# Between two layers of a fused kernel: the routing count, the sums and the list of places reordered, three lists moved behind a weight split, filler transposes added

## The reference

```
attn = softmax(scale * q @ k.T, blocks of 64 causal) @ v        # 4 batches, 8 heads, 576 positions, 64 wide
x    = elu(x @ w_in) @ w_out                                    # 512 -> 2048 -> 512
do_compute = x @ w_skip > 0                                     # the others leave the kernel as x
e_idx  = argmax(x @ w_gate)                                     # one expert of 8 for each token
gate_w = softmax(x @ w_gate)[e_idx]
out[do_compute] = x + gate_w * (relu(x @ w1[e_idx]) @ w2[e_idx])   # 512 -> 1024 -> 512
```

## Time and profile before

| | |
|---|---|
| median of three runs | 790.11 us |
| profiled execution, its own time | 791.72 us |
| its span | 789.9 us |
| TensorE busy | 758.0 us, 96% of the span |
| VectorE, ScalarE, GpSimd busy | 66%, 44%, 31% |
| the chain that ended last: TensorE, ScalarE, VectorE | 86%, 5%, 4% |
| mean granted TensorE clock | 0.993 of full |

### The profile page before, as it was taken

The page is one execution under the profiler, slowest core; times in us unless marked ns, Lnnn a source line. Parts: engine busy times, 40 slices in busy tenths (PEclk is TensorE's granted clock), DMA queues, the critical chain, the costliest instruction groups (busy, mean ns, idle before and its releaser), DMA issues.

```text
span 789.9 us, 15565 instructions
## 1 busy us (share of the span) xinstructions
PE 758.0 (96%) x5170; PEld 639.8 (81%) x5171; DVE 524.1 (66%) x1331; ACT 347.8 (44%) x830; POOL 245.3 (31%) x240
## 2 busy tenths in 40 slices
PE   5999999899999999999999999999987999999995
PEld 3777777688998888898988998888865777887884
DVE  3888888954337974984797598436665997367342
ACT  3888888644322213223222322324452774446231
POOL 4888887944501201210121021000112231222211
PEclk9999999999999999999999999999998999999998
DMA  9556677462422112101210200502424898174000
GB/s 163 133 149 157 163 162 188 144 198 61 147 79 103 48 57 91 50 21 62 59 41 0 90 22 27 214 0 81 135 95 126 270 340 303 46 229 153 34 15 9
DMA packets 101061, 88.15 MB, mean 112 GB/s; under 512 B 63812, under 2 KB 78532, under 8 KB 100880
## 3 DMA queue, kind: packets, MB, share of 16 engines
q1 hardware_dynamic: 95584, 81.89, 34.7%
q0 software_dynamic: 3056, 5.00, 1.9%
q10 hardware_dynamic: 2368, 0.59, 0.4%
HBM read 72.26 MB, written 18.34 MB: 115 GB/s over the span
## 4 chain that ended last, share of the span: by engine, by line
PE 86%; ACT 5%; DVE 4%; issue 3%; DVEq 1%; DMA 1%; POOL 0%; SPq 0%; ACTq 0%; POOLq 0%
PE h_ps L1733 12%; PE out_ps L1733 12%; PE h_ps L1734 12%; PE h_ps L1735 12%; PE out_ps L1735 11%; PE out_ps L1734 11%; PE o_ps L684 5%; PE s_ps L668 3%; ACT prob L541 3%; PE t_ps L593 2%; PE out_ps L1869 1%; PE s_ps L663 1%; ACT pt L525 1%; PE tr_ps L1834 1%; DMA raw_qk<-in_q_dram 1%
## 5 line engine op out<-in xcount | busy, mean ns | idle before, releaser
L1558 ACT ACTIVATE ex<-h_ps 128x384 f32<-128x384 f32 x96 | 47.3, 493 | 272.3 <-PE h_ps L1735 272.3
L1733 PE MATMUL h_ps<-xt_hi,wi_hi 128*128 128x384 f32 x384 | 131.8, 343 | 0.0
L1734 PE MATMUL h_ps<-xt_lo,wi_hi 128*128 128x384 f32 x384 | 129.7, 338 | 0.0
L1735 PE MATMUL h_ps<-xt_hi,wi_lo 128*128 128x384 f32 x384 | 129.7, 338 | 0.0
L1394 DVE TENSOR_SCALAR ex<-ex 128x384 f32<-128x384 f32 x96 | 36.9, 385 | 131.1 <-ACT ex L1558 129.7
L1733 PE MATMUL out_ps<-wo_hi,gt 128*128 128x512 f32 x288 | 114.5, 398 | 0.0
L1735 PE MATMUL out_ps<-wo_hi,gt 128*128 128x512 f32 x288 | 113.9, 396 | 0.0
L1734 PE MATMUL out_ps<-wo_lo,gt 128*128 128x512 f32 x288 | 113.3, 393 | 0.0
L541 ACT ACTIVATE prob<-s_ps,negmax 128x128 f32<-128x128 f32 (+2 forms) x144 | 77.8, 556 | 14.1 <-DVE negmax L399 13.7
L1276 DVE CUSTOM_DVE_ANT_0 x2t<-x,w_raw 128x512 bf16<-128x512 f32 x108 | 82.7, 806 | 0.4
L1172 POOL TENSOR_TENSOR xt_lo<-x_raw,xt_hi 128x384 fp32r<-128x384 f32 x20 | 28.3, 1413 | 157.8 <-ACT xt_hi L1575 157.5
(11 more groups left out here) (180 smaller groups left out, 1589.0 us busy)
## 6 DMA issues: line engine op xcount, KB each, us to landing
w_raw<-in_moe_w_dram SPq DMA_DIRECT2D x56, 512.0 KB, 5.2
raw_qk<-in_q_dram SPq DMA_DIRECT2D x32, 144.0 KB, 3.2
attn_t<-attn_sb SPq DMA_DIRECT2D x16, 288.0 KB, 2.2
x_raw<-attn_t SPq DMA_DIRECT2D x24, 192.0 KB, 2.4
w_raw<-recip_rows SPq DMA_DIRECT2D x48, 96.0 KB, 2.8
out_dram<-x SPq DMA_DIRECT2D x18, 256.0 KB, 2.1
x_rows<-x SPq DMA_DIRECT2D x18, 256.0 KB, 2.6
v<-in_v_dram SPq DMA_DIRECT2D x32, 128.0 KB, 2.9
```

The source lines that it names most:

```text
L1558: act.activation(ex[:, f % 2], h_ps[:, f % 2, 0:NB], ACT.Exp).then_inc(ex_done, 1)
L1733: pe.matmul(dst, stat[0], mov[0], start=start, stop=False, skip_group_check=True)
L1734: pe.matmul(dst, stat[0], mov[1], start=False, stop=False, skip_group_check=True)
L1735: return pe.matmul(dst, stat[1], mov[0], start=False, stop=stop, skip_group_check=True)
```

## The change

- `assign`: the wait for the softmax sum, `guarded` and the reciprocal move behind both steps of `whole`.
- ScalarE's `soften(LAST, 2)` moves ahead of `relu(0, 0)`.
- The count is issued after six of the twelve matmuls of `hidden(0, 0, 0, 1)`.
- Two steps that copied the count and added the early shift become one; `memset` and seven one-element sums become three sums of eight elements, over a zeroed and padded row `sums`.
- The four loads of `meta_sb` stand between the two `ht_low`.
- The lists of experts 5, 6 and 7 move behind `now(1)`, `xt_low(1)` and the four `w1_low`.
- The gathers of tiles 0 and 1 take their offsets from `tile_ids`; `gather_ids` is not written for them.
- TensorE: six of eight chunks of `output(0, 0)`, 18 transposes of the identity into `lg_ps` (which nobody reads any more), `turn_x(1)`, and then the other two chunks.

The core of the diff:

```diff
-        META_STEPS = 6 + E - 1
+        META_STEPS = 7
@@ gather
-                hold(pool, held)
-                pool.tensor_copy(gather_ids[:, :], tile_ids[:, bass.ds(t, 1)]).then_inc(gather_set, 1)
+                known = isinstance(t, int) and t < 2
+                if known:
+                    pool.sem_inc(gather_set, 1)
+                else:
+                    hold(pool, held)
+                    pool.tensor_copy(gather_ids[:, :], tile_ids[:, bass.ds(t, 1)]).then_inc(gather_set, 1)
...
+                ids = tile_ids[:, t:t + 1].bitcast(U32) if known else gather_ids[:, 0:1]
@@ VectorE, first(e, i, t, ask)
                     past(0)
-                    for j in range(HALVES):
-                        ht_low(0, j)
+                    ht_low(0, 0)
                     at = [0] + [tiles_of(dve, listing)[0] for listing in range(1, E // 2 + 1)]
+                    ht_low(0, 1)
                     dve.wait_ge(table_in, 16)
-                    for listing in range(E):
-                        list_tiles(listing, at[listing] if listing < len(at) else tiles_of(dve, listing)[0])
+                    for listing in range(len(at)):
+                        list_tiles(listing, at[listing])
                     now(1)
                     xt_low(1)
                     for j in range(PIECES):
                         w1_low(1, 1, j)
+                    for listing in range(len(at), E):
+                        list_tiles(listing, tiles_of(dve, listing)[0])
@@ VectorE, the sums
-            chain(dve.tensor_copy(more_f[:, :], cnt))
-            chain(dve.tensor_tensor(more_f[:, 0:1], more_f[:, 0:1], base_e[0:1, 0:1], ALU.add))
+            more = sums[:, 0, PAD + 1:PAD + 1 + E]
+            dve.wait_ge(sums_zeroed, 3)
+            chain(dve.tensor_tensor(more_f[:, :], cnt, early_row[:, :], ALU.add))
             chain(dve.tensor_tensor(over[:, :, :], more_f[:, :].unsqueeze(2).to_broadcast([1, E, NT]),
                                     bound[:, :].unsqueeze(1).to_broadcast([1, E, NT]), ALU.is_gt))
-            chain(dve.tensor_reduce(more_f[:, :], over[:, :, :], AX_X, ALU.add))
-            chain(dve.memset(before_f[:, 0:1], 0.0))
-            for e in range(1, E):
-                chain(dve.tensor_tensor(before_f[:, e:e + 1], before_f[:, e - 1:e],
-                                        more_f[:, e - 1:e], ALU.add))
+            chain(dve.tensor_reduce(more, over[:, :, :], AX_X, ALU.add))
+            for step_at, by in enumerate((1, 2, 4)):
...
+                chain(dve.tensor_tensor(dst, row_in[:, PAD:PAD + E], row_in[:, PAD - by:PAD - by + E], ALU.add))
@@ ScalarE
+            soften(LAST, 2)
             relu(0, 0)
-            soften(LAST, 2)
@@ TensorE, first(e, i, t, ask)
-                    output(0, 0, range(FCE))
+                    output(0, 0, range(FCE - 2))
+                    for c in range(WARM):
+                        pe.transpose(lg_ps[:, 0:P], ident[:, :], ident[:, :])
                     turn_x(1)
+                    output(0, 0, range(FCE - 2, FCE))
@@ TensorE, ahead of the experts
-            hidden(0, 0, 0, 1)
+            hidden(0, 0, 0, 1, [0, 1])
             count(NT, rk_done)
+            hidden(0, 0, 0, 1, [2, 3])
```

More of the change, by code:

```diff
@@ L768, in experts @@
     HALVES = FE // BANK
+    WARM = 18
     TURN_K = 2
@@ L894, in experts @@
         before_f = sb("before_f", [1, E], F32)
+        PAD = E // 2
+        sums = sb("sums", [1, 3, PAD + E + 1], F32)
+        early_row = sb("early_row", [1, E], F32)
         meta_sb = sb("meta_sb", [1, E], I32)
@@ L940, in experts @@
         early_in, early_listed = sem("early_in"), sem("early_listed")
+        sums_zeroed = sem("sums_zeroed")
         table_in = sem("table_in")
@@ L1190, in gather @@
                     pool.wait_ge(listed, lists)
-                hold(pool, held)
-                pool.tensor_copy(gather_ids[:, :], tile_ids[:, bass.ds(t, 1)]).then_inc(gather_set, 1)
+                known = isinstance(t, int) and t < 2
[4 more added lines that the diff above has]
+                    pool.tensor_copy(gather_ids[:, :], tile_ids[:, bass.ds(t, 1)]).then_inc(gather_set, 1)
                 if is_zero(t):
                     pool.wait_ge(in_zeroed, 1)
-                if isinstance(t, int) and t < 2:
+                if known:
                     for s in range(TB):
@@ L1200, in gather @@
                 rows = LAST * NB if is_zero(t) else N
+                ids = tile_ids[:, t:t + 1].bitcast(U32) if known else gather_ids[:, 0:1]
                 pool.indirect_dma_start(
-                    e_in, None, x2_rows[0:rows, :], bass.IndirectOffsetOnAxis(ap=gather_ids[:, 0:1], axis=0),
+                    e_in, None, x2_rows[0:rows, :], bass.IndirectOffsetOnAxis(ap=ids, axis=0),
                     bounds_check=rows - 1, oob_is_err=False).then_inc(gathered, 16)
@@ L1338, in assign @@
                                   chosen[:, :], ALU.add).then_inc(route, 1)
-                made(t, A_STEPS + 3)
+                made(t, A_STEPS + 2)
                 dve.tensor_scalar(whole[:, :], slot_f[:, :], 1.0 / P, 0.5 / P - 0.5, ALU.mult,
                                   ALU.add).then_inc(route, 1)
-                dve.reciprocal(entry[j][:, 1:2].bitcast(F32), guarded[:, :]).then_inc(route, 1)
-                made(t, A_STEPS + 5)
+                made(t, A_STEPS + 4)
                 dve.tensor_scalar(whole[:, :], whole[:, :], float(3 << 22), -float(3 << 22),
                                   ALU.add, ALU.add).then_inc(route, 1)
-                made(t, A_STEPS + 7)
+                dve.wait_ge(probs_done, t + 1)
+                dve.tensor_scalar(guarded[:, :], psum_row[:, :], 1e-9, None, ALU.add).then_inc(route, 1)
+                made(t, A_STEPS + 5)
                 dve.scalar_tensor_tensor(far[:, :], whole[:, :], 1.0 - P * COLS, far[:, :],
                                          ALU.mult, ALU.add).then_inc(route, 1)
-                made(t, A_STEPS + 8)
+                made(t, A_STEPS + 6)
+                dve.reciprocal(entry[j][:, 1:2].bitcast(F32), guarded[:, :]).then_inc(route, 1)
+                made(t, A_STEPS + 7)
                 dve.scalar_tensor_tensor(slot[j][:, :], slot_f[:, :], float(COLS), far[:, :],
@@ L1365, in early_shift @@
                 dve.tensor_scalar(base_e[:, 0:1], early_gap[:, :], 0.0, None, ALU.max).then_inc(early_base, 1)
+                dve.wait_ge(sums_zeroed, 2)
+                dve.tensor_scalar(early_row[:, 0:1], early_gap[0:1, :], 0.0, None, ALU.max)\
+                   .then_inc(sums_zeroed, 1)
             def list_early():
@@ L1408, in step @@
                         dve.wait_ge(stored, 16 * attend["pairs"] // 2)
+                    dve.memset(sums[:, :, :], 0.0).then_inc(sums_zeroed, 1)
+                    dve.memset(early_row[:, :], 0.0).then_inc(sums_zeroed, 1)
                     dve.memset(gw_past[:, :], 0.0).then_inc(final_done, 1)
@@ L1533, in chain @@
                 dve.wait_ge(route, at)
-            chain(dve.tensor_copy(more_f[:, :], cnt))
-            chain(dve.tensor_tensor(more_f[:, 0:1], more_f[:, 0:1], base_e[0:1, 0:1], ALU.add))
+            more = sums[:, 0, PAD + 1:PAD + 1 + E]
+            dve.wait_ge(sums_zeroed, 3)
+            chain(dve.tensor_tensor(more_f[:, :], cnt, early_row[:, :], ALU.add))
             chain(dve.tensor_tensor(over[:, :, :], more_f[:, :].unsqueeze(2).to_broadcast([1, E, NT]),
                                     bound[:, :].unsqueeze(1).to_broadcast([1, E, NT]), ALU.is_gt))
-            chain(dve.tensor_reduce(more_f[:, :], over[:, :, :], AX_X, ALU.add))
-            chain(dve.memset(before_f[:, 0:1], 0.0))
-            for e in range(1, E):
-                chain(dve.tensor_tensor(before_f[:, e:e + 1], before_f[:, e - 1:e],
-                                        more_f[:, e - 1:e], ALU.add))
-            chain(dve.scalar_tensor_tensor(meta_sb[:, :], before_f[:, :], float(META_BASE),
-                                           more_f[:, :], ALU.mult, ALU.add))
+            chain(dve.tensor_reduce(more, over[:, :, :], AX_X, ALU.add))
+            for step_at, by in enumerate((1, 2, 4)):
+                row_in = sums[:, step_at]
+                dst = sums[:, step_at + 1, PAD:PAD + E] if step_at < 2 else before_f[:, :]
+                chain(dve.tensor_tensor(dst, row_in[:, PAD:PAD + E], row_in[:, PAD - by:PAD - by + E], ALU.add))
+            chain(dve.scalar_tensor_tensor(meta_sb[:, :], before_f[:, :], float(META_BASE), more,
+                                           ALU.mult, ALU.add))
             over_experts(dve, first, other)
```

2 lines of the change are left out of this document (removed).

## The result

The changed kernel takes 793.48 us, the median of 20 runs (791.45 to 796.47), beside 791.25 for the kernel before over as many runs (789.47 to 792.76). The medians are 2.2 us apart. The changed kernel is slower. The forecast of 791.4 was too low by 2 us, though its range held. What came is the first rival: the slower one, with the clock.

The account below looks back on a forecast made before the run. The prediction took TensorE to bound the kernel, ending last for 86%. Of 4.7 us gained before tile 2's turn, VectorE's later rows leave 0.3: 791.72 minus 0.3 is 791.4, range 788.6 to 794.0.

Parts of the forecast that it names:

- the first rival: TensorE's new wait before tile 2's turn lets the clock fall; twelve matmuls cost 2.36 us more: 793.7; chance 0.25.
- the first output matmul: TensorE's first output matmul, waiting for `ht_lo`, starts at 587.1 instead of 589.03, nearly 2 us sooner.
- the first list: On VectorE, behind the moved loads: starts at 589.75 instead of 590.65, 0.9 us sooner.
- the gain stops at `now(2)`: VectorE's tile 2 rows, behind the moved lists, end at 607.5; of TensorE's 4.7 us gain, 0.3 are left.
- The GpSimd part: From list 1's end to tile 1's gather DMA: 1.0 us (0.8 to 1.2) without the ids copy, instead of 1.48.
- The three lists: Moved lists of experts 5, 6 and 7 with their loads, behind the `w1_low`: 2.6 us (1.6 to 3.8).
- The load and branch: On VectorE before `gw_past`: load for the number of tiles, arithmetic and branch, no longer hidden, 1.1 us (0 to 1.5).
- the row: On VectorE, from `gw_past` to the end of tile 2's `x_now`: 1.96 us.
- the reading of the three times: The kernel before's three run times say holes of this size aren't followed by a clock fall each time.
- harmless up to 2.50 us: TensorE's wait of about 2 us before tile 1's rows keeps full clock, being under the harmless 2.50.
- The second rival: Transposes before tile 1's turn do nothing for the clock; it falls there, yet the time is 791.6; chance 0.14.
- The third and fourth: Rivals: moved lists cost only 1.6 us, 789.3, chance 0.15; tile 1's gather lands at 2.1 or 5-plus us, 0.10.

Follow-up runs that it names:

- number 1: Changed kernel with all eight lists ahead of `x_now` of tile 1 again: 789.15 us, ratio to the kernel before 0.9983.
- number 3: Kernel before with one edit, the lists of experts 5, 6 and 7 moved behind the four `wi_lo`: 795.62 us, ratio 1.0053.
- number 4: Changed kernel with 34 more transposes filling TensorE's new wait before the turn of tile 2's rows: 791.84 us, ratio to the kernel before 1.0014.
- 8: Changed kernel with 17 matmuls of 512 columns filling the new wait before the turn of tile 2's rows: 792.40 us, ratio to the kernel before 1.0019.
- number 2: Changed kernel with lists 5 and 6 ahead of tile 1's `x_now` and list 7 right behind it, in VectorE's waits: 788.20 us, ratio to before 0.9969.
- 11: Kernel before with only the split output and the 18 transposes: 789.40 us, ratio 0.9989.
- 5: number 2 without the 18 transposes: 789.36 us, ratio to the kernel before 0.9985.
- number 6: number 2 with nine matmuls of 512 columns in place of the 18 transposes: 788.35 us, ratio to the kernel before 0.9971.
- 10: number 1 with the output whole ahead of the turn, no transposes, ids copied for all gathers: 790.26 us, ratio to the kernel before 0.9993.

## Why the prediction was right or wrong

**Right, step by step.** The count was expected at 583.6 and stands at 583.59; `x_past` 585.4 and 585.41; the first output matmul 587.1 and 587.25; the first list 589.75 and 589.81; tile 1's `x_now` 594.9 and 595.24, with VectorE idle for the gather before it; `hidden` 597.45 and 597.88, at full clock. The step on which the forecast stood, that the gain stops at `now(2)`, held: TensorE waits 4.18 us there, and numbers 1 and 3 show from both sides that the moved lists make that wait. The range held because it took in the first rival, which the prediction thought less likely than its forecast.

**A little small.** The GpSimd part took 1.20 us from list 1's end, not 1.0. The three lists took 2.83, not 2.6: the longer gap of 1.23 us ahead of one list, which the prediction had counted as a delay seen once, came again. The load and branch took 1.20, not 1.1, the row 2.01, not 1.96. With the last `wi_lo` ending 0.42 us later, most of it from the later `x_now`, they put the end of `now(2)` at 608.31, not 607.5, and the first output at 609.13, not 608.3. So instead of minus 0.3 the sum without any clock is plus 0.55.

**Wrong: the chance of the first rival.** The prediction gave 0.25 to the fall of the clock in the new wait, priced at 2.36 us. It fell in the profiled execution and in number 3's, the rest of the span then being 2.3 to 2.5 us longer, and in the profiles with the wait filled (4 and 8) it didn't fall there and all but 0.4 us of that time is gone. The mean clock of the changed kernel's 20 executions was 0.988 to 0.995, with none at the 0.997 and 0.998 that numbers 4 and 8 reach in some. It averages 0.992, as for the kernel before: the change took one fall away, ahead of tile 1, where its time would have gone into the wait for `now(2)` anyway, and put another where nothing hides it.

**Wrong: the reading of the three times.** The prediction took the two quicker runs of the kernel before for executions without a fall. Over the 81 executions of that kernel beside the experiments the mean clock is 0.989 to 0.993, never near 0.997, while its time spreads over 4 us. So the kernel before very likely loses clock in practically every execution, and the 1.6 us probably lay elsewhere: the last `ranks` matmul alone starts up to 2.4 us apart in the profiles of the different kernels. Against such a base the right sum was 0.55 for the first output matmul plus what the clock costs behind it. The prediction's 2.36 would make 2.9; in the profiled pair the part from that matmul to the end of the span grew from 181.3 to 183.5, by 2.15, which makes 2.7, the difference of the two spans. The ratio says 2.5. The forecast's "1.3 slower" was the sum of a wrong base and a missing fall.

**Wrong: harmless up to 2.50 us.** The prediction called the hole before tile 1's rows safe since the clock had been full behind one of 2.50. One execution can't show that: the clock fell behind 1.98 us in number 2 and behind that very hole of 2.50 in numbers 3 and 11. Nor does length alone decide: it stayed full behind 3.00 us in number 1.

**The second rival fell.** The Trainium skill ("TensorE: Matmul & The Clock Gate", the section on transposes) says that transpose mode "doesn't count as PE-busy the same way". Numbers 2, 5 and 6 disagree: 18 transposes raise the mean clock from 0.9915 to 0.9949 and take 1.2 us off, about what matmuls of the same length do; here the measurement decides. That a fall ahead of tile 1 would cost nothing in the changed kernel fits the record, though: number 4's profile has one, 0.50 from 598 to 601, and TensorE was through with its matmuls of tile 1 at 605.9 even so, 3.1 us before `x_now` was done at 609.0.

**The third and fourth.** Cheap lists did not come (2.83 us, beside 1.6). Tile 1's gather landed in 3.3 us again.

## What to carry to other kernels

Work that is moved out of one wait needs another wait to go into: find in the timeline who next waits for the engine, and put the work into that engine's own idle stretches (2.98 and 1.38 us of VectorE here) rather than behind its longest instructions. A new hole on TensorE is priced with the clock behind it: here the late turn alone cost 0.6 us against the kernel before, and the clock 2.15 more. Whether an idle stretch costs the clock can't be read off one execution. The mean clocks of many executions say more, but they count every fall of the span: all profiles here have one behind TensorE's last matmul, and four (the changed kernel, 2, 8 and 11) have one near 25 us.

## What the runs showed of the hardware

Falls of the clock from 1.00 to 0.50 came behind holes of 1.94 us (number 6), 1.98 (2), 2.09 (4), 2.50 (3 and 11), 2.70 (before), 3.64 (10), 4.08 (5) and 4.2 us (the changed kernel and 3), and in other executions not behind holes of 2.04 (the changed kernel), 2.13 (8), 2.50 (before) and 3.00 us (1). One, in number 2, came with no hole longer than 0.3 us since 575. Fillers that do no useful work, transposes or matmuls, into a PSUM bank nobody reads, paid for themselves ahead of tile 1 (1.2 us between the medians of 5 and 2). What decides in which execution it falls isn't settled here.
